# W3 in an attention and two-MLP kernel: four of eight tiles turned by VectorE in blocks of 32, another head, masks ahead of weights

## What is computed

```python
# attention, for each batch and head
q_assign = argmax(q_n @ c_n.T); k_assign = argmax(k_n @ c_n.T)      # 16 clusters
scores = where(q_assign == k_assign, scale * q @ k.T, -1e9)
x = softmax(scores) @ v                                             # to 1536 x 512
# first network, d_ff 2048
h = x @ w_in; P = a0 + a1 h + a2 h^2 + a3 h^3; Q = 1 + |b0||h| + |b1| h^2
x = (P / (Q + 1e-6)) @ w_out                                        # 1536 x 512
# second network, d_ff 1024
out = ((x @ w1) * (x @ w2)) @ w3 @ w_out2                           # 1536 x 512
```

## Time and profile before

| | |
|---|---|
| median of 3 runs | 739.5 us (739.35 to 740.12) |
| profiled execution | 741.63 us, its span 739.8 us |
| TensorE busy | 726.2 us, 98% of the span |
| VectorE, ScalarE, GpSimd busy | 536.5, 433.0, 356.8 us |
| mean granted clock of TensorE | 0.991 |
| issues of W3 | 8 loads of 512 KB, 3.7 us to landing |

### The profile page before, as it was taken

The page is one execution under the profiler, slowest core; times in us unless marked ns, Lnnn a source line. Parts: engine busy times, 40 slices in busy tenths (PEclk is TensorE's granted clock), DMA queues, the critical chain, the costliest instruction groups (busy, mean ns, idle before and its releaser), DMA issues.

```text
span 739.8 us, 13271 instructions
## 1 busy us (share of the span) xinstructions
PE 726.2 (98%) x5057; PEld 605.2 (82%) x5057; DVE 536.5 (73%) x863; ACT 433.0 (59%) x770; POOL 356.8 (48%) x266
## 2 busy tenths in 40 slices
PE   7899999999999999999999999999999999999998
PEld 6667777777767788888888888887889999999898
DVE  7888888888864577768677686775876656577983
ACT  4366667766656788877676676774443233234542
POOL 5068788787785646752222223440204466653032
PEclk9699999999999999999999999999999999999999
DMA  8234555545421352000000021103100110100111
GB/s 170 57 94 127 142 126 140 152 115 149 106 64 34 111 163 77 1 0 1 1 0 2 1 97 53 79 5 109 58 29 19 39 30 29 29 0 16 43 58 58
DMA packets 67023, 47.79 MB, mean 65 GB/s; under 512 B 30544, under 2 KB 59408, under 8 KB 66960
## 3 DMA queue, kind: packets, MB, share of 16 engines
q1 hardware_dynamic: 66960, 46.95, 23.1%
HBM read 28.35 MB, written 3.15 MB: 43 GB/s over the span
## 4 chain that ended last, share of the span: by engine, by line
PE 94%; DVE 3%; ACT 1%; DMA 1%; issue 1%; SPq 0%; POOL 0%; DVEq 0%; ACTq 0%
PE psum L1449 92%; PE psum L1454 1%; PE psum L769 1%; DVE psum L1978 1%; DVE OPS L1913 1%; DMA RAWQK<-in_k 0%; DMA BQS<-NMT 0%; DVE MROW L1978 0%; ACT P L1756 0%; PE psum L1527 0%; POOL G L573 0%; DVE psum L1946 0%; ACT OPS L1732 0%; ACT BQS L1732 0%; ACT OPS L1720 0%
## 5 line engine op out<-in xcount | busy, mean ns | idle before, releaser
L573 POOL TENSOR_TENSOR G<-TT,G 128x512 fp32r<-128x512 f32 x47 | 61.1, 1299 | 150.1 <-ACT G L452 150.1
L2143 POOL TENSOR_TENSOR PSUMS<-PSUMS,P 128x768 f32<-128x768 f32 x64 | 108.1, 1689 | 17.1 <-ACT P L1756 9.4
L1756 ACT ACTIVATE P<-psum 128x768 f32<-128x768 f32 x96 | 76.3, 809 | 47.5 <-PE psum L1449 47.2
L1978 DVE TENSOR_REDUCE psum<-psum 128x1 f32<-128x768 f32 x90 | 86.3, 959 | 20.9 <-PE psum L1449 19.9
L1449 PE MATMUL psum<-G,WSPLIT 128*128 128x512 f32 x360 | 86.8, 390 | 0.2 <-POOL G L573 0.2
L1449 PE MATMUL psum<-XT,WSPLIT 128*128 128x512 f32 x360 | 86.5, 389 | 0.0
L500 DVE SCALAR_TENSOR_TENSOR HH<-UU,ABSB,psum 128x512 f32<-128x512 f32 x48 | 35.9, 748 | 69.0 <-ACT TT L430 69.0
L1449 PEld LDWEIGHTS psum<-G,WSPLIT 128*128 128x128 f32 x360 | 67.3, 188 | 15.1 <-POOL G L573 0.9
L1449 PEld LDWEIGHTS psum<-XT,WSPLIT 128*128 128x128 f32 x360 | 67.6, 188 | 14.0
L1449 PE MATMUL psum<-P,V 128*32 128x194 f32 x1536 | 76.0, 332 | 0.1
L1449 PE MATMUL psum<-XT,SW 128*128 128x384 f32 x384 | 71.7, 334 | 0.0
(11 more groups left out here) (169 smaller groups left out, 1511.3 us busy)
## 6 DMA issues: line engine op xcount, KB each, us to landing
W3R<-in_moe_w SPq DMA_DIRECT2D x8, 512.0 KB, 3.7
RAWF<-in_moe_w SPq DMA_DIRECT2D x16, 256.0 KB, 3.2
RAWQK<-in_q SPq DMA_DIRECT2D x16, 192.0 KB, 3.2
RAWQK<-in_k SPq DMA_DIRECT2D x16, 192.0 KB, 3.7
BQS<-OPS SPq DMA_DIRECT2D x16, 192.0 KB, 2.8
OPS<-OPS SPq DMA_DIRECT2D x16, 192.0 KB, 3.0
V<-in_v SPq DMA_DIRECT2D x16, 192.0 KB, 2.7
XT<-XH SPq DMA_DIRECT2D x64, 48.0 KB, 2.0
```

Of the source, the lines that this page charges most:

```text
L573: nc.gpsimd.tensor_tensor(G[:, n % 2, 1, :], TT[:, n % 4, :], G[:, n % 2, 0, :].bitcast(F32), ALU.subtract).then_inc(g_lo, 1)
L1756: nc.scalar.activation(P32[:, (2 * u + n) % 4, :, 0:QS].rearrange("p (x y) n -> p x y n", x=2), score_banks(u, n).rearrange("p x (y n) -> ...
L1978: nc.vector.tensor_reduce(rows[:, n:n + 1], maxima_banks(u, n), AX.XY, ALU.max).then_inc(sm_free, 1)
L2143: nc.gpsimd.tensor_tensor(total, P32[:, (2 * u) % 4, :, 0:QS] if n == 1 else total, P32[:, (2 * u + n) % 4, :, 0:QS], ALU.add).then_inc(p_ ...
```

## The change

**Turned by VectorE.** Of the 16 halves of W3, those from 2 to 9 (tiles 1 to 4) are no longer turned by TensorE. VectorE's transpose turns blocks of 32 by 32, so SP now loads these tiles with their blocks already in place (`load_blocks`, four loads of 32 partitions with pieces of 1 KB), and `turn_w3` writes the turned half to a new tile W3T in SBUF, of which `round_w3` and `w3_rest` read. For this the columns of W3 are taken in another order of contraction; W4 is loaded in the same order by four loads, and the tiles that TensorE still turns (0, 5, 6, 7) are loaded by `load_plain`, in pieces of 32 floats. The later tiles wait for `w3_turned` instead of `ft_ready`. Halves 2, 3, 4 are turned at the end of the passes n = 45, 46, 47 of the rational loop, halves 5, 6, 7 before the last `y_rest`, halves 8 and 9 at n = 3 and 4 of the fold stage. `SUMS_STEP` has another table.

**Head.** k of unit 0 is issued by ScalarE instead of SP. `keep_busy` has more dummies, `score_max(0, 3)` to `(0, 5)` stand before `sides(3)`.

**Masks.** In the attention steps SP places the masks before it loads weights.

```diff
@@ rational_scalar, rational_vector
-                act.wait_ge(ld_w4, 16)
+                act.wait_ge(ld_w4, 64)
...
                 quotient(dve, n - 1)
+                if n >= LAST - 3:
+                    turn_w3(dve, n - LAST + 5)
             cubic_end(dve, LAST - 1)
...
             for n in range(2):
                 w3_rest(dve, n)
+            for n in range(5, 8):
+                turn_w3(dve, n)
             y_rest(NCH - 1)
@@ later_loads
+        TURNED = range(2, 10)
...
-            sp.dma_start(W4RAW[:, 0], w4.rearrange("(j p) m -> p j m", p=P)).then_inc(ld_w4, 16)
+            for g in range(4):
+                sp.dma_start(W4RAW[g * QUAD:(g + 1) * QUAD, 0],
+                             w4[g * 2 * P:(g + 1) * 2 * P].rearrange("(j c) m -> c j m", c=QUAD)).then_inc(ld_w4, 16)
+
+            def load_plain(i):
+                for g in range(4):
+                    sp.dma_start(W3R[:, i % 4, :].rearrange("p (j x c) -> p j x c", x=4, c=QUAD)[:, :, g, :],
+                                 w3[i * P:(i + 1) * P, g * 2 * P:(g + 1) * 2 * P].rearrange("p (j c) -> p j c", c=QUAD)).then_inc(ld_w3[i % 4], 16)
+
+            def load_blocks(i):
+                for g in range(4):
+                    sp.dma_start(W3R[g * QUAD:(g + 1) * QUAD, i % 4, :].rearrange("p (x n) -> p x n", x=4),
+                                 w3[i * P:(i + 1) * P, g * 2 * P:(g + 1) * 2 * P].rearrange("(x r) n -> r x n", x=4)).then_inc(ld_w3[i % 4], 16)
+
             sp.wait_ge(out_done, 2 * NF + 6)
-            for i in range(4):
-                sp.dma_start(W3R[:, i, :], w3[i * P:(i + 1) * P, :]).then_inc(ld_w3[i], 16)
+            for i in range(1, 4):
+                load_blocks(i)
+            load_plain(0)
...
             for i in range(4, 8):
-                sp.wait_ge(ft_ready, 2 * (i - 4) + 2)
-                sp.dma_start(W3R[:, i % 4, :], w3[i * P:(i + 1) * P, :]).then_inc(ld_w3[i % 4], 16)
+                if i == 4:
+                    sp.wait_ge(ft_ready, 2)
+                    load_blocks(i)
+                else:
+                    sp.wait_ge(w3_turned, 2 * (i - 4))
+                    load_plain(i)
                 if i == 4:
                     load_pair(0)
                     load_pair(1)
@@ fold stage
-        SUMS_STEP = (0, 0, 2, 3, 1, 2, 1, 1, 1, 3, 1, 3, 2, 3, 2, 3)
+        SUMS_STEP = (0, 0, 1, 2, 1, 1, 1, 1, 2, 3, 2, 3, 2, 3, 1, 5)
...
+        def w3_part(n):
+
+            return W3T[:, (n - 2) // 4, 4 + (n - 2) % 4, :] if n in TURNED else psum[:, n % 2, :]
+
+        def turn_w3(dve, n):
+
+            i, half = n // 2, n % 2
+            dve.wait_ge(ld_w3[i % 4], 64 * (i // 4 + 1))
+            dve.wait_ge(out_done, 2 * NF + (8 if n < 6 else 10))
+            nc.vector.transpose(w3_part(n).rearrange("p (j x r) -> p j x r", j=4, x=4),
+                                W3R[:, i % 4, :].rearrange("p (x j c) -> p j x c", x=4, j=8)[:, 4 * half:4 * half + 4]).then_inc(w3_turned, 1)
...
-            nc.scalar.copy(WT[:, n % 2, 0, :], psum[:, n % 2, :]).then_inc(ft_hi, 1)
+            nc.scalar.copy(WT[:, n % 2, 0, :], w3_part(n)).then_inc(ft_hi, 1)
...
             for n in range(FOLDS):
                 fold(n)
-                if n + 2 < FOLDS:
+                if TURNED.stop <= n + 2 < FOLDS:
                     transpose_w3(pe, n + 2)
...
                     fold_rest(dve, n // 2 - 1)
+                if n in (3, 4):
+                    turn_w3(dve, n + 5)
@@ sync, step(u)
                     load_qk(u + 5)
+                if has(u + 3):
+                    place_masks(u + 3)
                 if u % 2 == 1 and u < 2 * EARLY_W - 2:
                     load_weights(sp, (u + 1) // 2, ld_w[(u + 1) // 2])
-                if has(u + 3):
-                    place_masks(u + 3)
@@ scalar
             nc.scalar.preload_act_table_set("natural_log_exp_and_others")
+            nc.scalar.dma_start(RAWQK[:, 0, :, 1, :], k[0, 0].rearrange("(p n) d -> p n d", p=P)).then_inc(ld_qk[0], 16)
```

More of the change, by code:

```diff
@@ L141, in build @@
             W4RAW = ph("W4RAW", [P, 2, NF2, DM], F32)
+            ph("GAP_W3", [P, 4, FF2], F32)
+            W3T = ph("W3T", [P, 2, NF2, DM], F32)
         with ExitStack() as phase:
@@ L255, in build @@
         y_sum_lo = sem("y_sum_lo")
+        w3_turned = sem("w3_turned")
         ft_ready = sem("ft_ready")
@@ L762, in transpose_w3 @@
             if half == 0:
-                pe.wait_ge(ld_w3[i % 4], 16 * (i // 4 + 1))
+                pe.wait_ge(ld_w3[i % 4], 64 * (i // 4 + 1))
             if n < 2:
@@ L771, in transpose_w3 @@
             last.then_inc(ft_ready, 1)
+        def w3_part(n):
[6 more added lines that the diff above has]
+                                W3R[:, i % 4, :].rearrange("p (x j c) -> p j x c", x=4, j=8)[:, 4 * half:4 * half + 4]).then_inc(w3_turned, 1)
         def round_w3(act, n):
-            act.wait_ge(ft_ready, n + 1)
+            if n in TURNED:
+                act.wait_ge(w3_turned, n - 1)
+            else:
+                act.wait_ge(ft_ready, n + 1 if n < 2 else n - 7)
             if n >= 2:
                 act.wait_ge(fold_done, n - 1)
-            nc.scalar.copy(WT[:, n % 2, 0, :], psum[:, n % 2, :]).then_inc(ft_hi, 1)
+            nc.scalar.copy(WT[:, n % 2, 0, :], w3_part(n)).then_inc(ft_hi, 1)
         def w3_rest(dve, n):
@@ L784, in w3_rest @@
                 dve.wait_ge(g_lo, LAST - 3)
-            nc.vector.tensor_tensor(WT[:, n % 2, 1, :], psum[:, n % 2, :], WT[:, n % 2, 0, :].bitcast(F32),
+            nc.vector.tensor_tensor(WT[:, n % 2, 1, :], w3_part(n), WT[:, n % 2, 0, :].bitcast(F32),
                                     ALU.subtract).then_inc(ft_free, 1)
@@ L1391, in _ @@
             sp.dma_start(CEN, centroids.rearrange("h c d -> (h c) d")).then_inc(ld_cen, 16)
-            load_qk(0)
+            sp.dma_start(RAWQK[:, 0, :, 0, :], q[0, 0].rearrange("(p n) d -> p n d", p=P)).then_inc(ld_qk[0], 16)
             load_qk(1)
@@ L1606, in _ @@
             similarities(1)
-            keep_busy(3, 8)
+            keep_busy(3, 14)
             score_max(0, 0)
             similarities(2)
+            keep_busy(1, 2)
             score_max(0, 1)
+            keep_busy(1, 2)
             score_max(0, 2)
+            keep_busy(1, 2)
+            score_max(0, 3)
+            keep_busy(1, 2)
+            score_max(0, 4)
+            keep_busy(1, 2)
+            score_max(0, 5)
             sides(3)
-            score_max(0, 3)
-            score_max(0, 4)
-            score_max(0, 5)
             turn_maxima(0)
@@ L1618, in _ @@
             pe.wait_ge(sims_read, 3)
-            keep_busy(6, 5)
+            keep_busy(6, 6)
             score_max(1, 1)
```

## The result

The changed kernel takes 743.28 us (median of 6 runs, 742.7 to 743.87), the kernel before 739.49 in the same set (6 runs, 739.35 to 740.52). The ratio is 1.0046, with a 95% interval of 1.0036 to 1.0057: slower by 3.8 us on the medians, where 3.6 us faster was forecast. The profiled execution took 743.87 us, its span is 742.1.

A forecast was written before the change was run, and what follows sets the result against it. TensorE, busy 98% of the span, was taken as the bound. Head -2.3, rational end +0.65, transposes -3.5 and fold waits +1.5 summed to -3.6, giving 735.9 us; range 733.8 to 738.6.

The forecast's parts named there:

- The fold stage, what is late next: fold 7: Fold stage: VectorE's remainder, stretched beside GpSimd to about 1.6 us, makes TensorE wait 1.4 us; all fold waits together +1.5.
- Fold 11: Fold stage: one item more of 0.47 us behind `pair_last` gives a wait of 0.1 us.
- Folds 5 and 15: Fold stage: waits of 0.4 us at the first and 0.2 at the second, where the latter had 0.58.
- The gain: Fold stage: TensorE loses 8 groups of four transposes at 0.44 us, -3.5 us; exactly six groups stay between the folds.
- The end of the rational stage: End of the rational loop: half 4's block transpose stands in the chain to the last G, +0.65 us, from 0 to 1.3.
- Block transposes: VectorE's transposes of 512 elements from SBUF: 0.73 us long, 0.65 from start to start; over 1 us would show it wrong.
- The transfers: Loads of W3 and W4: tiles in 128-byte pieces take 5 us each and arrive before they are needed, so free.
- rival 2: Fold stage: small pieces arrive late; at 60 ns per packet tile 7 is 10 us late, total +6, 745.5 us; chance 0.06.
- Masks: Attention steps: placing masks before weights on SP's queue changes nothing, zero, bounds one issue of 0.65 us either way.
- The head: Start of the kernel: three edits bring the first exponential 2.3 us earlier, -2.3, bounds 0.7 to 3.0 gained.
- the order of `score_max`: Head: `score_max` 3 to 5 before unit 3's transposes close VectorE's gaps of 0.46 and 0.24 us, 0.7 us gained.
- rival 1: Head: the clock falls all the same; whole change -2.0, 737.5 us, chance 0.22; falling at 18 us, 739.8, chance 0.08.

The follow-up runs named there:

- the run with the pieces: Changed kernel with GpSimd's first two fold-stage subtractions in six pieces of 256 elements: 738.73 us, ratio 0.9982 to the kernel before.
- masks alone: Kernel before with only the masks placed ahead of the weights on SP's queue: 740.05 us, ratio 1.000 to the kernel before.
- head alone: Kernel before with the change's head edits and mask order, nothing of W3: 738.41 us, ratio 0.9973 to the kernel before.

## Why the prediction was wrong

- **The fold stage, what is late next: fold 7.** This step failed. I had the right two operands, the right place and the right instruction, but read the 1.38 us of `TX<-YS,TX` as a factor of two and a half. It is a hold until GpSimd's instruction ends: 0.96 us of it left, and 0.42. A factor gives one operation 1.6 us; a hold gives it whatever is left of 2.4 us. I also looked at WT alone, where `YS<-XT` one step ahead met the first instruction and WT the second: 2.2 and 1.1 us over their length. The wait was 3.44, not 1.4. GpSimd's instruction also began 18.9 us into the folds, 1.8 earlier than before (527.54 against 506.89), because the folds ahead of it had become shorter; I kept its old distance.
- **Not in the sum at all: the clock in the folds.** +2.8 us. I asked about the clock in the head only. A wait that I had at 1.4 us would not have brought it down: the run with the pieces waited 1.28 us at 1.00.
- **Fold 11**: 0.63 us where 0.1 was forecast. GpSimd's third instruction (542.79, 0.89 us) meets a `YS<-YS` that takes 0.97. Before, `WT<-psum,WT` stood beside it and took 0.69. Folds 5 and 15: 0.34 and 0.20, forecast 0.4 and 0.2.
- **The gain**, -3.5: right, six groups stay. The **breaks** I had left out, +0.5 by the remainder.
- **The end of the rational stage**, +0.65: +0.6, and it goes when half 4 leaves the chain. **Block transposes**: 0.70 us, forecast 0.73; three in 1.89.
- **The transfers**, rival 2: free. In the 25 us from 505 on, the first row below (packets, MB, share of 16 engines, as in the earlier trace rows) has 14592 packets, mean 180 bytes, at 14.9 ns each, less than the 19.7 of before; no fold waits for a DMA. The small pieces do cost the DMA engines time: 12 bytes per ns of an engine, where before's four loads of W3 (the second row, from the 20 us from 455 on, in pieces of 4 KB) moved 22. Nothing waited for that. The page DMA: Bandwidth & Descriptors of the Trainium skill (Specifications) says that transfers below 512 bytes are read, modified and written; the lower rate fits, and no run here tells whether that is its cause.

```profile
q1 hardware_dynamic: 14592, 2.62, 54.5%
...
q1 hardware_dynamic: 576, 2.10, 29.9%
```

- **Masks**, 0: shown by their run.
- **The head**, -2.3: 2.0 alone, some 0.5 in the changed kernel. The 0.7 of it that I gave to the order of `score_max` was no gain of that order: at the full clock the gaps are not there (masks alone). No run takes the head's edits one by one; the profiles show its gain where the clock holds past 26 us, with the first exponential at 28.83 (head alone) against 30.40. The gaps between 23 and 28.7 us that I named for rival 1 are what the clock fell after. And the profile that I measured from was that of an execution with a costly head: 741.6 us, 2.1 above the median. The masks' profile, with the same head, has its first exponential 1.7 us earlier. Such executions are the fewer: of 110 of the kernel before listed beside these runs, 26 have a mean granted clock of 0.990 or 0.991 as that profile has, and their median is 1.2 us above that of the 80 at 0.997 and more. I carried that difference along as a constant; it sat in the very stage that I priced.

Put together against the medians: folds +3.8, rational +0.6, head -0.6 as the remainder: +3.8. The error of the forecast, 7.4 us, is 5.8 in the folds (2.0 fold 7, 0.5 fold 11, 0.5 breaks, 2.8 clock) and the rest in the head.

## What to carry to other kernels

Before an operand of VectorE moves from PSUM to SBUF, list the GpSimd instructions that can run beside it: from then on it waits for the end of any that began first, and so does everything queued behind it. Keep GpSimd's instructions short where VectorE feeds TensorE; the same work in pieces took GpSimd longer and the kernel 4.7 us less. And price a wait of TensorE twice, once for itself and once for the clock: in the folds, where TensorE was full between its waits, waits up to 1.9 us left it alone, and one of 3.44 cost 2.8 us more. In the head of the changed kernel the clock fell behind gaps of only 0.74 and 0.58 us, so the length of one wait doesn't settle it.

## What the runs showed of the hardware that I had not expected

- A held operation ends 0.42 us (384 elements) or 0.54 us (512) after GpSimd's instruction, which is less than its 0.55 and 0.69 alone.
- Idle stretches of TensorE and the clock after them, in the folds: 1.28, 1.91 us: 1.00. 2.38 us: 1.00 in one profile, and after 2.36 in another 0.83, 0.50 and 0.82 in the three windows. 3.25 and 3.44: half. Ten dummies inside 3.4 us were enough to hold it. The kernels with waits near 2.4 us spread over 3.1 and 4.3 us (740.31 to 743.45, 739.21 to 743.54), the one with pieces alone over 2.4.
- Behind the same wait of 3.44 us the half clock cost 2.8 us in one kernel and 1.6 in another.
- The granted clock is shown as 1.00 from the start, but the ten first dummies take 4.06 to 4.64 us where fourteen later ones take 3.39: 0.4 to 0.46 us each, then 0.24. Five dummies at a granted clock of a half took 2.34 us, 0.47 each (masks alone, 26.22): the first ones run near that pace, and the clock shown doesn't say so.
- ScalarE's DMA issue runs beside its own table load (0.78 us, the load from 0.75 to 2.03).
